# Decay tables as single-pass products over 128 rows, small tables in one load, and tile 0's first layer in another order

## The reference

```python
for t in range(S):                                   # attention, gamma per head
    state = gamma[None, :, None, None] * state + np.einsum('bhd,bhe->bhde', k[:, :, t], v[:, :, t])
    y[:, :, t] = scale * np.einsum('bhd,bhde->bhe', q[:, :, t], state)
...
h = np.maximum(x @ w_in, 0.0)                        # layer 1: 512 -> 2048 -> 512
x = h * h @ w_out
...
rms = np.sqrt(np.mean(x * x, axis=-1, keepdims=True) + 1e-06)
xn = x / rms * rms_g                                 # layer 2: 512 -> 1536 (twice) -> 512
g = xn @ w_gate
return (g * (1.0 / (1.0 + np.exp(-g)))) * (xn @ w_val) @ w_out
```

## Time and profile before

| | us |
|---|---|
| median of 3 runs | 1084.7 |
| lowest, highest | 1083.77, 1084.81 |
| the profiled execution | 1083.67 |
| its span | 1081.9 |
| PE busy in it | 1075.2 |
| DVE, ACT, POOL busy | 857.6, 625.9, 334.4 |

### The profile page before, as it was taken

How to read it: one execution, slowest core, us unless ns; L and a number is a source line. 1 busy time by engine, 2 the same in 40 slices (tenths; PEclk the granted TensorE clock), 3 DMA queues, 4 the chain that set the end, 5 groups by cost and what they waited for, 6 DMA issues and landing times.

```text
span 1081.9 us, 16680 instructions
## 1 busy us (share of the span) xinstructions
PE 1075.2 (99%) x6466; PEld 920.4 (85%) x6466; DVE 857.6 (79%) x916; ACT 625.9 (58%) x934; POOL 334.4 (31%) x242
## 2 busy tenths in 40 slices
PE   9999999999999999999999999999999999999998
PEld 7888788888888888888888888998888998888898
DVE  4685899878879878789899988878675976867684
ACT  3786676466765667664664545646454555544453
POOL 2664552004450005430034653005444002544000
PEclk9999999999999999999999999999999999999999
DMA  9999648763447645365742336653114563120355
GB/s 339 354 403 413 231 172 288 239 215 117 172 159 238 213 153 173 139 237 196 225 145 95 121 113 234 195 176 99 39 64 158 197 208 114 41 77 1 117 184 187
DMA packets 68173, 195.80 MB, mean 181 GB/s; under 512 B 7672, under 2 KB 22136, under 8 KB 63232
## 3 DMA queue, kind: packets, MB, share of 16 engines
q1 hardware_dynamic: 65344, 190.42, 50.6%
q10 hardware_dynamic: 2752, 4.33, 1.1%
HBM read 152.18 MB, written 42.48 MB: 180 GB/s over the span
## 4 chain that ended last, share of the span: by engine, by line
PE 93%; ACT 2%; DMA 2%; issue 1%; DVE 1%; SPq 0%; ACTq 0%; POOL 0%; DVEq 0%
PE Y L811 13%; PE Y L812 13%; PE Y L813 13%; PE Z L811 8%; PE X L811 8%; PE X L812 8%; PE Z L812 8%; PE Z L813 8%; PE X L813 8%; DMA item_scratch<-ops 1%; PE Z L761 1%; PE Z L751 1%; ACT k_dec L926 1%; PE Y L736 1%; PE R L781 1%
## 5 line engine op out<-in xcount | busy, mean ns | idle before, releaser
L660 POOL TENSOR_TENSOR w_ops<-raw_w,w_ops 128x512 fp32r<-128x512 f32 x90 | 128.4, 1426 | 504.4 <-ACT w_ops L938 504.3
L998 ACT CAST ops<-hid 128x1024 fp32r<-128x1024 f32 x147 | 154.0, 1048 | 159.9 <-PE Z L813 55.8
L1355 DVE TENSOR_TENSOR ops<-hid,ops 128x1024 fp32r<-128x1024 f32 x147 | 180.4, 1227 | 51.4 <-ACT ops L998 50.7
L660 POOL TENSOR_TENSOR w_ops<-sums_w,w_ops 128x512 fp32r<-128x512 f32 x120 | 169.1, 1412 | 122.0 <-ACT w_ops L938 121.6
L811 PE MATMUL Y<-ops,w_ops 128*128 128x512 f32 x360 | 140.5, 390 | 1.4 <-DVE hid L1551 0.9
L812 PE MATMUL Y<-ops,w_ops 128*128 128x512 f32 x360 | 140.1, 389 | 0.0
L813 PE MATMUL Y<-ops,w_ops 128*128 128x512 f32 x360 | 140.1, 389 | 0.0
L811 PE MATMUL Y<-ops 128*128 128x256 f32 (+1 forms) x360 | 117.1, 325 | 0.0
L812 PE MATMUL Y<-ops 128*128 128x256 f32 (+1 forms) x360 | 117.1, 325 | 0.0
L813 PE MATMUL Y<-ops 128*128 128x256 f32 (+1 forms) x360 | 117.1, 325 | 0.0
L1037 ACT ACTIVATE gt<-gt 128x512 f32<-128x512 f32 x72 | 45.1, 633 | 118.6 <-DVE gt L1613 41.0
(11 more groups left out here) (167 smaller groups left out, 2464.1 us busy)
## 6 DMA issues: line engine op xcount, KB each, us to landing
ops<-item_scratch SPq DMA_DIRECT2D x147, 512.0 KB, 4.1
raw_w<-w_f SPq DMA_DIRECT2D x30, 1024.0 KB, 4.9
item_scratch<-hid SPq DMA_DIRECT2D x30, 512.0 KB, 3.1
qk_sb<-qkv SPq DMA_DIRECT2D x24, 512.0 KB, 7.9
kv_sb<-qkv SPq DMA_DIRECT2D x20, 512.0 KB, 8.8
y_scratch<-hid SPq DMA_DIRECT2D x12, 512.0 KB, 6.0
raw<-y_scratch SPq DMA_DIRECT2D x3, 2048.0 KB, 10.7
raw<-w_b SPq DMA_DIRECT2D x5, 1024.0 KB, 5.0
```

The lines of the kernel that those rows point to most:

```text
L660: nc.gpsimd.tensor_tensor(w_ops[:, k, 1], front_w_source(m, k), f32(w_ops[:, k, 0]), ALU.subtract).then_inc(w_lo, 1)
L998: nc.scalar.copy(hop_at(n)[:, 0], hid[:, 2 * g:2 * g + 2, OPERAND[k], :]).then_inc(hop_hi, 1)
L1355: nc.vector.tensor_tensor(hop[:, 1], hid[:, 2 * g:2 * g + 2, OPERAND[k], :], f32(hop[:, 0]), ALU.subtract).then_inc(hop_lo, 1)
```

## The change

1. `decay_rows` becomes 32 rows: each factor is split in a leading and a trailing part of 12 mantissa bits, and the rows of leading x leading, leading x trailing and trailing x leading stand under each other (24 rows, and 8 of zeros). They land in `y_sb`, ACT casts them to fp32r in `spare`, DVE fills rows 32 to 127 with zeros, and `rows_times` is a single pass over 128 rows. PE waits for both casts. All three products stand ahead of `scores(0)`.
2. `zeros(5)` becomes `zeros(8)`.
3. `causal`, `decay_k` and `decay_s` become one array, `tables`, with one DMA, behind `decay_rows` on ACT's queue. DVE, POOL and ACT wait for it.
4. SP stores items 4 and 5 ahead of 0 and 1, and 2 and 3 behind 11.
5. In run 0 ACT's `seed` stands ahead of `high_front(0, 3)`.
6. In runs 1 to 3 units 6 and 7 (and those that answer to them in run 2) move from slots 3 and 4 to slot 5, which DVE now has, behind its `relu_square`.

```diff
@@ units_at
-        first, count = ((0, 0), (0, 1), (1, 3), (4, 3), (7, 1), (8, 0), (8, 0))[slot]
+        first, count = ((0, 0), (0, 1), (1, 3), (4, 2), (6, 0), (6, 2), (8, 0))[slot]
@@ build
-        causal_sb = sb("causal_sb", [P, P], scope=att)
-        decay_s_sb = sb("decay_s_sb", [P, CH, PAIRS], scope=att)
-        decay_k_sb = sb("decay_k_sb", [P, CH, H], scope=att)
+        tables_sb = sb("tables_sb", [P, CH * (H + PAIRS) + P], scope=att)
...
-        rows_sb = y_sb[0:H].rearrange("p a b -> p (a b)")[:, 0:DM + 3 * P]
+        staged_rows = y_sb[:].rearrange("p a b -> p (a b)")[:, 0:DM + 3 * P]
+        rows_sb = spare[:, 0].rearrange("p l n -> p (l n)")[:, 0:DM + 3 * P]
@@ SP
-            for i in range(14):
+            for i in (4, 5, 0, 1, 6, 7, 8, 9, 10, 11, 2, 3, 12, 13):
                 store_item(*divmod(i, 7))
@@ POOL
-            pool.wait_ge(decay_k_loaded, 16)
+            pool.wait_ge(tables_loaded, 16)
@@ PE
             pe.wait_ge(zeroed, 1)
-            zeros(5)
-            pe.wait_ge(rows_loaded, 16)
+            zeros(8)
+            pe.wait_ge(rows_set, 1)
+            pe.wait_ge(rows_padded, 1)
             rows_times(Z[:, 0, :], 0)
             rows_times(Z[:, 1, :], 1).then_inc(mask_made, 1)
+            rows_times(decay_q_ps, 2).then_inc(decay_placed, 1)
             scores(0)
-            rows_times(decay_q_ps, 2).then_inc(decay_placed, 1)
             scores(1)
@@ ACT, front_run
-                prep(0)
-                seed(run)
+                if run == 0:
+                    seed(run)
+                    prep(0)
+                else:
+                    prep(0)
+                    seed(run)
@@ ACT, start
-            act.dma_start(rows_sb, decay_rows).then_inc(rows_loaded, 16)
-            act.dma_start(causal_sb[:], causal).then_inc(causal_loaded, 16)
-            act.dma_start(decay_k_sb[:], decay_k).then_inc(decay_k_loaded, 16)
-            act.dma_start(decay_s_sb[:], decay_s).then_inc(decay_s_loaded, 16)
+            act.dma_start(staged_rows[0:4 * H], decay_rows).then_inc(rows_loaded, 16)
+            act.dma_start(tables_sb[:], tables).then_inc(tables_loaded, 16)
             act.wait_ge(consts_set, 1)
             nc.scalar.activation(warm[:], eps[:], ACT.Copy)
-            act.wait_ge(decay_k_loaded, 16)
+            act.wait_ge(rows_loaded, 16)
+            nc.scalar.copy(rows_sb[0:4 * H], staged_rows[0:4 * H]).then_inc(rows_set, 1)
+            act.wait_ge(tables_loaded, 16)
@@ DVE, start
-            dve.wait_ge(causal_loaded, 16)
+            dve.wait_ge(zeroed, 1)
+            for lo, hi in ((32, 64), (64, P)):
+                op = nc.vector.tensor_copy(rows_sb[lo:hi].rearrange("p (a b) -> p a b", b=P),
+                                           y_sb[lo:hi, 2, 0:P].unsqueeze(1).to_broadcast([hi - lo, 7, P]))
+            op.then_inc(rows_padded, 1)
+            dve.wait_ge(tables_loaded, 16)
             dve.wait_ge(mask_made, 1)
@@ DVE, front1_run
                 relu_square(p, Bb, z_taken, run + 1, h_b)
+                prep(m, 5, fresh, t)
```

More of the change, by code:

```diff
@@ L117, in units_at, with build @@
     return [(quads[i // 11], i % 11) for i in range(x, x + count) if 0 <= i < 11 * len(quads)]
-def build(nc, qkv, decay_rows, causal, decay_s, decay_k, w_f1, w_f2, w_b, rms_g, out):
+def build(nc, qkv, decay_rows, tables, w_f1, w_f2, w_b, rms_g, out):
     x_dram = nc.dram_tensor("x_scratch", (16, P, 2, 2, P), F32, kind="Internal").ap()
@@ L157, in build @@
         rows_loaded = sem("rows_loaded")
-        causal_loaded = sem("causal_loaded")
+        tables_loaded = sem("tables_loaded")
+        rows_padded = sem("rows_padded")
+        rows_set = sem("rows_set")
         mask_made = sem("mask_made")
         mask_set = sem("mask_set")
-        decay_k_loaded = sem("decay_k_loaded")
-        decay_s_loaded = sem("decay_s_loaded")
         k_first = sem("k_first")
@@ L257, in build @@
         decay_q_ps = R[:, 1, :]
-        rows_sb = y_sb[0:H].rearrange("p a b -> p (a b)")[:, 0:DM + 3 * P]
+        staged_rows = y_sb[:].rearrange("p a b -> p (a b)")[:, 0:DM + 3 * P]
+        rows_sb = spare[:, 0].rearrange("p l n -> p (l n)")[:, 0:DM + 3 * P]
+        decay_k_sb = tables_sb[:, 0:CH * H].rearrange("p (c h) -> p c h", c=CH)
+        decay_s_sb = tables_sb[:, CH * H:CH * (H + PAIRS)].rearrange("p (c a) -> p c a", c=CH)
+        causal_sb = tables_sb[:, CH * (H + PAIRS):]
         QT, KT = range(2)
@@ L791, in rows_times @@
             def rows_times(dst, i):
-                return nc.tensor.matmul(dst, rows_sb[:, DM + P * i:DM + P * i + P], rows_sb[:, 0:DM], start=True, stop=True)
+                return nc.tensor.matmul(dst, rows_sb[:, DM + P * i:DM + P * i + P],
+                                        rows_sb[:, 0:DM], start=True, stop=True)
             pe.wait_ge(zeroed, 1)
-            zeros(5)
-            pe.wait_ge(rows_loaded, 16)
+            zeros(8)
+            pe.wait_ge(rows_set, 1)
+            pe.wait_ge(rows_padded, 1)
             rows_times(Z[:, 0, :], 0)
             rows_times(Z[:, 1, :], 1).then_inc(mask_made, 1)
+            rows_times(decay_q_ps, 2).then_inc(decay_placed, 1)
             scores(0)
-            rows_times(decay_q_ps, 2).then_inc(decay_placed, 1)
             scores(1)
@@ L1323, in _ @@
                                              Z[:, i, :].rearrange("p (a t) -> p a t", a=PAIRS),
[L1324 removed]
+                                             causal_sb.unsqueeze(1).to_broadcast([P, PAIRS, P]), ALU.mult)
             op.then_inc(mask_set, 1)
@@ L1703, in decay_tables @@
     back = gamma[:, None] ** -t
-    rows = np.concatenate([forward.reshape(H, DM), back * (h % 2 == 0), back * (h % 2 == 1), 1.0 * (t // D == h % 2)], axis=1)
+    moving = halves(forward.reshape(H, DM))
+    held = halves(np.concatenate([back * (h % 2 == 0), back * (h % 2 == 1), 1.0 * (t // D == h % 2)], axis=1))
+    rows = np.zeros((4 * H, DM + 3 * P))
+    for i, (a, b) in enumerate(((0, 0), (0, 1), (1, 0))):
+        rows[H * i:H * i + H] = np.concatenate([moving[b], held[a]], axis=1)
     causal = 1.0 * (t >= np.arange(P)[:, None])
@@ L1708, in decay_tables, with halves, leading @@
     k = gamma[None, None, :] ** (S // 2 - np.arange(S).reshape(CH, P).T[:, :, None])
-    return [np.ascontiguousarray(a.astype(np.float32)) for a in (rows, causal, s, k)]
+    tables = np.concatenate([k.reshape(P, CH * H), s.reshape(P, CH * PAIRS), causal], axis=1)
+    return [np.ascontiguousarray(a.astype(np.float32)) for a in (rows, tables)]
+def halves(a):
+    def leading(x):
+        bits = np.ascontiguousarray(x.astype(np.float32)).view(np.uint32).astype(np.uint64)
+        return (((bits + 0x800) >> 12) << 12).astype(np.uint32).view(np.float32).astype(np.float64)
+    hi = leading(a)
+    return hi, leading(a - hi)
 def kernel(q, k, v, moe_w_in, moe_w_out, moe2_w_gate, moe2_w_val, moe2_w_out, moe2_rms_g):
@@ L1735 @@
     qkv = np.stack([feature_major(q), feature_major(k), token_major(k), token_major(v)], axis=3)
-    decay_rows, causal, decay_s, decay_k = decay_tables()
+    decay_rows, tables = decay_tables()
     arrays = {
@@ L1739 @@
         "decay_rows": decay_rows,
-        "causal": causal,
-        "decay_s": decay_s,
-        "decay_k": decay_k,
+        "tables": tables,
         "w_f1": front_blocks([moe_w_in], R1, 2),
```

1 line of the change is left out of this document (removed).

## The result

| | before | after |
|---|---|---|
| median, us (6 runs each) | 1084.74 | 1080.07 |
| lowest, highest | 1083.77, 1084.99 | 1079.79, 1081.49 |
| the profiled execution | 1083.67 | 1081.38 |
| its span | 1081.9 | 1079.5 |
| PE busy in it | 1075.2 | 1070.0 |

The ratio is 0.9961, with an interval of 0.9949 to 0.9974: 4.7 us less, 0.3 from the forecast. The missing part has a place in the trace. The six executions of after stand in two groups, four at 1079.8 to 1080.2 and two at 1081.4 to 1081.5, and the traced one belongs to the second. The mean granted clock that is on record for each execution tells the two groups apart as well: 0.998 of full speed in the two long ones, 0.999 to 1.000 in the four others.

The account below looks back on a forecast made before the run. The layers were taken as a chain of PE passes. Gains 2.7 (start) + 1.0 (run 0) + 1.2 (run 1) = 4.9 off the profiled 1083.67 gave 1078.8, as a median 1079.8; range 1077.6 to 1082.4.

Parts of the forecast that it names:

- the step to the median: Whole kernel: the profiled execution of before lies 1.0 under its median, so 1078.8 becomes 1079.8 for a median.
- Start, what PE does: Kernel start: zeros end at 4.95, three single table passes at 5.7 to 6.3; added waits cost nothing to 0.3.
- Start, the rise of the clock: Kernel start: passes over 128 rows lift PE's clock by about 6 us, where before it rose about 15.
- rises no earlier: Rival at the start: the clock's rise stays put, the start gains 1.8, 4.0 in all, 1080.7; chance 0.2.
- Start, what is late next: Kernel start: masks wait for `tables`, landing at 7.0; first state passes at 12.1 against 16.74, a gain of 4.6.
- What the DMAs give back: Attention: loads bind by chunk 17, margin 0.7 plus 2.5 of holes; 2.7 of the start's 4.6 is kept.
- The prediction's own sign of being wrong: Attention: the prediction called itself wrong if PE loses no time there; it expected load waits around chunks 9 to 11 and 17.
- the DMAs keep up: Rival in attention: loads give nothing back, 4.6 for the start, 6.8 in all, 1077.9; chance 0.17.
- The fall of the clock: Rival: PE idles from 8.5 to 9.6 for the first mask, the clock falls back, kernel slower; chance 0.04.
- Run 0: Tile 0, run 0: waits for the seed and `u2_saved` go, a gain of 1.0, bounds 0.4 to 1.0.
- Late next is DVE's `c22_done`: Tile 0, run 0: would be 0.3 in time; if DVE does not gain, up to 0.6 comes back.
- Run 1: Tile 0, run 1: product 6's wait for `c22_done` goes with the moved items, gaining 1.2, at least 0.8.

Follow-up runs that it names:

- zeros5: The changed kernel with `zeros(5)` in place of `zeros(8)`; 1080.41 us, ratio 0.996 to before.
- start_only: The kernel before with parts 1 to 3 of the change alone (stores, seed and units as before); 1080.95 us, ratio 0.9967.
- zeros8_8rows: The kernel before with `zeros(8)` in place of `zeros(5)` and nothing else, tables still over 8 rows in six passes; 1082.82 us, ratio 0.9981.
- rows32: The changed kernel with the table products over the 32 rows that hold data instead of 128; 1079.77 us, ratio 0.9956 to before.
- the run alone: Under run 0: parts 4 and 5 alone on before, 1085.09 us, ratio 1.0005. Under run 1: part 6 alone on before, 1083.39 us, ratio 0.9988.
- slots_only: The kernel before with part 6 alone (two units moved to slot 5); 1083.39 us, ratio 0.9988.

## Why the prediction was right, and where it was not

The total, 1079.8 against 1080.07, is right by luck: two of its terms were off by 2 us in opposite directions (1.9 for the loads, 2.0 for run 0), and two smaller errors, at the start and in the step to the median, made up the rest.

- **Start, what PE does.** Right. The zeros and the cast end within 0.7 of each other; the wait for the cast is 0.69, where "nothing to 0.3" was said, since `decay_rows` landed at 4.5 and not with ACT's table load. It costs nothing, as zeros5 showed with 1.87.
- **Start, the rise of the clock.** The forecast held for the kernel: up at about 5 in after, at about 4 in start_only. The part that the reason gave to the padded tables is not borne out: in both the clock rose before the table products began (5.52 and 5.57), in zeros8_8rows at 4 too, behind 16 passes of zeros where before has 10, and in rows32 it rose at 10.5 with no pass over 128 rows since 4.84. rows32 and zeros5 rose later and lost nothing. The rival "rises no earlier" priced a thing that, with the tables moved ahead of the scores, hardly sets the time.
- **Start, what is late next.** Right in kind, the masks behind `tables`. The array landed at 7.6 to 7.8, not at 7.0, and the state passes then come at 12.9 to 13.2, where the clock stays up: up to 3.8, not 4.6. The date of 7.0 was taken from the array's place in the queue, but the load ahead of it had grown from 28 to 112 KB, which the prediction does not mention (in after it landed after 3.8 us, and the array's 100 KB after 6.6). That this made it late is argued, not tested.
- **What the DMAs give back.** The step that failed. 1.9 us were taken off for loads that bind by chunk 17. In start_only, 3.8 earlier, nothing was lost, and in zeros8_8rows, 4.55 earlier, 0.4. The prediction's own sign of being wrong, that PE loses no time in attention, came true. The share of busy time was read as fullness; the engines moved 394 GB/s at a share of 1.01 where they had moved 367 at 0.99, so the share hid most of the room. Why it reads near 1 with that room is open. The rival "the DMAs keep up" was the case, at 0.17; its time, 1077.9, was not reached because of run 0 and the later array.
- **The fall of the clock.** Named as a rival, with its place (PE's pause) and 0.04, and ruled out by the steady state of the attention loop. It happens in some executions; in the traced one it lasted 3.4 us, not whole chunks, and cost 1.5: no reversal.
- **Run 0.** Also failed: +1.0 said, 1.0 lost in the traces and 0.6 in the run alone (interval -0.4 to +1.6). Both waits went as the steps said. "Late next is DVE's `c22_done`" was right too, but its date was worked out with DVE's operations at their old durations. The prediction followed what stands behind the moved instructions on ACT and SP, and not POOL, whose low parts follow ACT's casts: the combination, 1.22 before, took 2.32.
- **Run 1.** Right: 1.16 in the traces and 1.1 in the run alone, for 1.2.

So start +3.8 for 2.7 (3.6 in after, if the 1.5 of the fallen clock is added to its 2.05), run 0 -1.0 for +1.0, run 1 +1.2 for 1.2: 4.0 for 4.9, counted from the profiled execution, or 1079.7. The prediction then added 1.0 for the distance between before's trace and its median. After's median stands only 0.4 over 1079.7, so most of that distance did not carry over. A sum 0.9 too large and a shift 0.6 too large made the total come out right. Where before's 1.0 lies is not settled; the trace of slots_only, with the start of before, the clock up some 2 us later than there and layer 1 begun 1.05 later (94.01 for 92.96), suggests the start.

## What to carry to other kernels

When a wait is taken off an engine, follow what that engine feeds as well, and look at which engine pairs will then run side by side: here ACT's freed casts started POOL 1.1 us earlier in DVE's chain and turned a gain of 1 into a loss of 1, and one added wait on POOL gave about 2 back. A DMA share near 1 is no proof that earlier issues bring nothing; look at the rate beside it, and compare issue, landing and use of single loads in a kernel that issues them earlier. At a start, move the first thing that the steady loop waits for, and see what lands behind it in the same queues.

## What the runs showed of the hardware

- A DVE operation with two SBUF inputs beside POOL's took 2.32 instead of 1.22 (1024 columns) and 1.78 instead of 0.68 (512): 1.1 more each. Other operations met POOL for less of their time and took less (1.51 and 1.75 for 1024 columns in before's run 0). POOL's 512 columns took 1.31 alone and 2.13 beside it.
- The clock fell to its lower level (0.62 mean over 12 to 16) after a single pause of PE of 2.0 us, when PE had been at work again for 1.1. In another execution it did not fall after one of 1.75. Of the 12 executions of the two kernels with this pause 4 have a mean granted clock of 0.998, of 23 with the pause filled none is below 0.999.
- The clock's rise comes at different times with the same start: slots_only, whose start is that of before, had it up only at 17.5 and before at 15. With 16 passes of zeros instead of 10 (zeros8_8rows) it rose at 4 in the traced execution, and by the granted clock on record (0.995 to 0.998) it fell back in seven of the other nine. The times of that kernel spread over 5.7 us, where before's spread over 1.2 to 3.1 in the four comparisons.
- A DMA load (chunk 17's) issued 3.8 us earlier landed 4.4 earlier, at a share of 0.99 and then 1.01 over 4 to 64 us, while the rate rose from 367 to 394 GB/s.
